# Routed experts in slots of 256 rows, the first product with standing weights

## The chip, the cores and the metric

The kernel runs on one core of a Trainium2 chip. The metric is the device time of one execution, in microseconds, as the median of three executions. A core has five instruction streams that run side by side and meet at semaphores: TensorE (PE in the profile; its weight loads are shown apart as PEld), VectorE (DVE), ScalarE (ACT), GpSimd (POOL) and SyncE (SP, which only issues DMAs here). "Product" below means a chain of matmuls that add up in one place of PSUM, TensorE's result memory of eight banks.

## What is computed

Three stages follow one another: attention whose keys and queries must share a hash bucket, a gated feed-forward layer, and a layer of eight experts of which every row uses one. The change touches the third:

```python
N, D, E, F = (1536, 512, 8, 1024)
logits = x @ w_gate
e_idx = np.argmax(logits, axis=1)
...
for e in range(E):
    mask = e_idx == e
    ...
    h = np.maximum(x[mask] @ w1[e], 0.0)
    ye = h @ w2[e]
    out[mask] = gate_w[mask, None] * eom[mask, e, None] * ye
```

The inputs are drawn from a fixed seed. Counted with the reference on seed 0, the eight experts get 175, 179, 189, 226, 155, 205, 226 and 181 rows.

## The kernel before

All products are made of fp32r matmuls (float32 data in TensorE's faster format) on operands split in a high and a low part: high x high, high x low and low x high are added up, three matmuls for each block of 128 in the contraction. A matmul has a standing operand, 128 x 128, which a weight load puts into the array, and a moving operand, here of up to 512 columns, which streams through.

**Up to the experts** nothing is in another place after the change: attention by pairs of heads, the gated layer (L923), its output projection (L1059, twelve row tiles of 128) and, between the tiles' matmuls, the routing: logits, the chosen expert, the rank of each row among those of its expert, and the row's destination `dest`. POOL scatters each tile of `x2` with an indirect DMA (L797) into a DRAM scratch `routed`, in which two experts share a region and fill it from both ends. The scratch is filled with empty rows beforehand by `fill`, 52 DMAs of 257 KB from SP's queue.

**Slots.** The expert stage works through up to 19 slots of 128 rows (`SLOTS`); 12 are certain (`USED`), the others are run or skipped by a branch on the table entry `in_use`. Which expert a slot belongs to, where its rows lie (`tile_i`), when an expert's weights must be split (`wanted`) and on which of two sides of `expert_w` they lie (`expert_side`) stand in tables that DVE works out after the last tile (L1750 to L1791), and that the engines read with TENSOR_LOAD (`entry`, L350).

**One slot on TensorE** (`step` of the tensor block): `up_half` twice (L1109), each a product of 12 matmuls in which the turned rows `rowsT_h`, `rowsT_l` stand and 512 columns of the weights `w1_h`, `w1_l` move, so that the hidden rows come out with rows on the partitions. DVE applies the relu (L1797) and puts them in `hid`. For the second product the hidden values must have their columns on the partitions, so TensorE turns `hid` in two halves of four 128 x 128 transposes (`turn_hid`, L1120), ACT rounds them to the high part `hidT_h` (L1372) and DVE makes the low part `hidT_l` (L1809). `down` (L1129) is 24 matmuls in two halves, `hidT` standing and 512 columns of `w2` moving. The second product of slot s-1 runs behind the first product of slot s, with the turns between its halves. The next slot's rows (`rows_in`, 257 KB, loaded on ACT's queue at L1360) are turned in the same place (`turn_rows`, L1093), rounded by ACT (L1366) and split by DVE (L1802). `rows_done` (L1380) scales the finished rows into `rows_out`, and POOL stores them to their place in the output with an indirect DMA (L805).

**Weights.** Each expert's 4 MB come in four pieces of 1 MB (`load_piece`, SP's queue, L545 and L548). ACT writes the high part (L1348) and DVE the low part (L1654) of each piece into the side of `expert_w` that is not in use; a piece buffer is loaded again when its low part is done.

**Before the first slot** PE runs `keep_warm` (transposes of the identity into an idle bank, L985) while it waits for the scattered rows.

Of the kernel before, what the change touches and what calls it, by code (L numbers as in the profile page):

```python
# [17 lines left out]
P128 = 128  # L18
# [14 lines left out]
def build(nc, q, k, v, proj, w_gate, w_val, w_out, rms_g, router, out_gate, w1, w2, out):  # L33
# [22 lines left out]
    SLOTS = (N - (E - 1)) // P128 + 1 + (E - 1)  # L56
    USED = -(-N // P128)
    PIECE = C * FE // 2
    ROW = DM + 2
    REGION = NT + 1  # L60
    TILES = E // 2 * REGION
    FILLS = 8
    assert 6 * FILLS < TILES < 7 * FILLS
# [9 lines left out]
    routed_v = routed.rearrange("(s p) n -> p s n", p=P128)  # L73

# [3 lines left out]
    with ExitStack() as ctx:  # L78
# [31 lines left out]
        slot_i = at("slot_i", [P128, SLOTS], I32)  # L110
        slot_f = at("slot_f", [P128, SLOTS], F32)
# [17 lines left out]
        full_at = at("full_at", [1, NT], F32)  # L129
        over = at("over", [1, E, NT], F32)  # L130
        ends = [at(f"ends{i}", [1, 2 * E], F32) for i in range(4)]
        total_i = at("total_i", [1, 3], I32)
        past = at("past", [1, SLOTS, E], F32)
        before_e = at("before_e", [1, SLOTS, E], F32)
        expert_f = at("expert_f", [1, SLOTS], F32)
        expert = at("expert", [1, SLOTS], I32)
        expert_side = at("expert_side", [1, SLOTS], I32)
        odd = at("odd", [1, SLOTS], I32)
        odd_f = at("odd_f", [1, SLOTS], F32)
        nth = at("nth", [1, SLOTS], F32)  # L140
        tile_f = at("tile_f", [1, SLOTS], F32)
        tile_i = at("tile_i", [1, SLOTS], I32)
        change = at("change", [1, SLOTS], F32)
        wanted = at("wanted", [1, SLOTS], I32)
        in_use = at("in_use", [1, SLOTS + 1], I32)
        ended = at("ended", [1, SLOTS + 1], I32)
        stores = at("stores", [1, 2], I32)
        wanted_side = at("wanted_side", [1, SLOTS], I32)
# [100 lines left out]
        hid = at("hid", [P128, FE], F32, offset=addr[0] - 2 * C * P128 * 4)  # L249
        rows_in = [None] * 3 + [at("rows_in3", [P128, ROW], F32)]  # L250
        assert addr[0] <= x2_offset
        addr[0] = xT_offset + 4 * C * FE * 4
        for i in range(3):
            rows_in[i] = at(f"rows_in{i}", [P128, ROW], F32)
        assert addr[0] <= hT_offset - 3 * PIECE * 4
        addr[0] = hT_offset - 3 * PIECE * 4
        for i in range(3):
            piece[i] = at(f"piece{i}", [P128, PIECE], F32)
        addr[0] = x2_offset
        hidT_h = [at(f"hidT_h{i}", [P128, CF, P128], F32R) for i in range(2)]  # L260
        hidT_l = [at(f"hidT_l{i}", [P128, CF, P128], F32R) for i in range(2)]
        rowsT_h = at("rowsT_h", [P128, C, P128], F32R)
        rowsT_l = at("rowsT_l", [P128, C, P128], F32R)
        rows_out = [at(f"rows_out{i}", [P128, DM], F32) for i in range(2)]
# [10 lines left out]
                 "half_ready x_done pool_passed sp_passed "  # L275
# [3 lines left out]
                 "table_made scattered w1_high w2_high w1_low w2_low rows_turned rowsT_high rowsT_low hid_made relu_made hid_turned "  # L279
                 "hidT_high hidT_low "  # L280
                 "out_made outs_ready slots_done").split()
# [4 lines left out]
         half_ready, x_done, pool_passed, sp_passed,  # L286
# [5 lines left out]
         relu_made, hid_turned, hidT_high, hidT_low,  # L292
         out_made, outs_ready, slots_done) = (sems[n] for n in names)
# [58 lines left out]
        def if_used(eng, s_, body):  # L352

            if s_ < USED:
                body()
            elif s_ < SLOTS:
                used = entry(eng, in_use, s_, 1)
                with eng.If(used != 0):
                    body()

        def if_ended(eng, s_, body):

            if s_ >= USED:
                with eng.If(entry(eng, ended, s_, 1) != 0):
                    body()

        def where_wanted(eng, s_, split):

            e = entry(eng, wanted, s_, E - 1)
            with eng.If(e != 0):  # L370
                split(e, entry(eng, wanted_side, s_, 1))
# [1489 lines left out]
```

## Time and profile before

| | |
|---|---|
| median of 3 runs | 803.07 us (802.38 to 803.78) |
| profiled execution | 803.83 us, of it 801.9 us are the span of the trace |
| PE busy | 772.8 us, 96% of the span |
| DVE, ACT, POOL busy | 504.0, 375.3, 317.5 us |
| expert stage, first matmul of the first product to the last scaling of rows | 587.94 to 794.66 us |

Times in the trace are microseconds from the start of the span. A group of instructions is shown as line, engine, operation, out<-in by the program's names, and a count. In square brackets stands how long the engine was idle before it and what ended that. The chain of waits is the work that ended last, followed back from the end: each piece of it is released by the one before. A matmul's shown duration reaches beyond the start of the next one, because they are pipelined; how fast they follow one another is read from the starts, or from a piece of the chain divided by its count.

### The profile page before, as it was taken

The page shows a single profiled execution, that of the slowest core. Times are in us where ns is not written, and L with a number is a line of the kernel's source. Part 1 is how long each engine was busy: PE and PEld are TensorE (multiplying, and loading weights), DVE is VectorE, ACT ScalarE, POOL GpSimd, SP SyncE. Part 2 cuts the span into 40 slices and gives each one's busy share as a digit, 9 for nine tenths or more (in the row PEclk, how much of TensorE's full clock was granted, in tenths as well). Part 3 has the DMA queues.
Part 4 walks back from the last instruction along what each step waited for, and adds up shares of the span by engine and source line. Part 5 has one row for each costly group of instructions (what it writes and reads, how often), then busy time and mean ns, then how long its engine had stood idle before and what let it go on. Part 6 is the DMA issues. An engine that isn't in the chain of part 4 may idle for free.

```text
span 801.9 us, 14327 instructions
## 1 busy us (share of the span) xinstructions
PE 772.8 (96%) x4294; PEld 685.5 (85%) x4294; DVE 504.0 (63%) x983; ACT 375.3 (47%) x672; POOL 317.5 (40%) x340
## 2 busy tenths in 40 slices
PE   7999999999999899999999999999889999999995
PEld 5899889988888899999999988888768888777774
DVE  7999999999987544334343533464673647655640
ACT  5888888888886111110111234434423524553331
POOL 7877777788888353244222001111200201010110
PEclk9999999999999899999999999999999999999999
DMA  6898769657302231112110131031544466454410
GB/s 199 235 236 215 205 166 281 178 142 167 84 2 60 64 89 40 39 39 60 58 39 0 39 121 38 27 132 45 178 146 145 151 228 243 150 203 173 145 47 22
DMA packets 53717, 96.84 MB, mean 121 GB/s; under 512 B 6841, under 2 KB 21189, under 8 KB 53656
## 3 DMA queue, kind: packets, MB, share of 16 engines
q1 hardware_dynamic: 48648, 84.90, 35.7%
q10 hardware_dynamic: 2768, 4.87, 2.3%
q0 software_dynamic: 2240, 6.31, 2.0%
q8 instruction: 32, 0.52, 0.3%
q14 instruction: 29, 0.24, 0.1%
HBM read 58.51 MB, written 21.04 MB: 99 GB/s over the span
## 4 chain that ended last, share of the span: by engine, by line
PE 83%; DVE 10%; issue 3%; ACT 2%; POOL 1%; DMA 1%; ACTq 0%; POOLq 0%; DVEq 0%
PE ps_t L1059 13%; PE ps_s L923 12%; PE ps_t L1129 11%; PE ps_s L1109 11%; PE ps_t L923 6%; PE ps_t L876 6%; DVE pT_l L1483 3%; PE ps_o L923 3%; PE ps_p L923 3%; PE ps_s L862 3%; PE ps_s L863 3%; DVE negmax L1465 2%; PE ps_s L1120 2%; PE ps_o L891 1%; PE ps_o L893 1%
## 5 line engine op out<-in xcount | busy, mean ns | idle before, releaser
L697 POOL TENSOR_SCALAR probs<-probs,rden,alone 128x768 f32<-128x768 f32 x96 | 93.5, 987 | 35.6 <-DVE rden L1477 35.6
L1483 DVE TENSOR_TENSOR pT_l<-ps_t,pT_h 128x384 fp32r<-128x384 f32 x192 | 97.5, 548 | 5.6 <-ACT pT_h L1219 4.6
L805 POOL DMA_INDIRECT out_dram<-rows_out,rows_in x16 | 23.0, 1440 | 193.9 <-ACT rows_out L1380 183.9
L923 PE MATMUL ps_s<-xn,w_h 128*128 128x384 f32 x384 | 97.4, 334 | 0.0
L1209 ACT ACTIVATE probs<-ps_s,negmax 128x768 f32<-128x768 f32 x96 | 87.0, 906 | 19.2 <-DVE negmax L1465 18.5
L1465 DVE TENSOR_REDUCE negmax<-ps_s 128x1 f32<-128x770 f32 x96 | 90.8, 947 | 3.8 <-PE ps_s L863 3.0
L1219 ACT ACTIVATE pT_h<-ps_t 128x384 fp32r<-128x384 f32 x192 | 85.2, 491 | 16.6 <-PE ps_t L876 15.5
L1654 DVE TENSOR_TENSOR expert_w<-piece,expert_w 128x2048 f32 (+1 forms) x32 | 72.1, 2288 | 31.7 <-ACT expert_w L1348 26.4
L876 PE MATMUL ps_t<-ident,probs 128*128 128x128 f32 x576 | 87.4, 282 | 4.5 <-DVE pT_l L1483 2.4
L1109 PE MATMUL ps_s<-expert_w,rowsT_h 128*128 (+1 forms) x256 | 81.9, 401 | 2.7 <-issue 1.6
L1129 PE MATMUL ps_t<-expert_w,hidT_h 128*128 (+1 forms) x256 | 82.1, 402 | 2.2 <-DVE hidT_l L1809 1.4
L876 PEld LDWEIGHTS ps_t<-ident,probs 128*128 128x128 f32 x576 | 63.2, 140 | 24.0 <-DVE pT_l L1483 9.7
L797 POOL DMA_INDIRECT routed<-x,dest x12 | 21.0, 1754 | 128.4 <-DVE x L1732 128.4
L923 PEld LDWEIGHTS ps_s<-xn,w_h 128*128 128x128 f32 x384 | 69.4, 188 | 0.0
L862 PE MATMUL ps_s<-k_a,q_a 128*128 128x384 f32 x192 | 65.8, 343 | 3.5 <-ACT probs L1209 2.1
L1348 ACT ACTIVATE expert_w<-piece 128x2048 f32 (+1 forms) x32 | 59.6, 1907 | 17.4 <-issue 17.4
L1372 ACT ACTIVATE hidT_h<-ps_s 128x512 fp32r<-128x512 f32 x32 | 19.0, 594 | 101.6 <-PE ps_s L1120 73.3
L863 PE MATMUL ps_s<-k_b,q_b 128*128 128x384 f32 x192 | 65.5, 341 | 0.0
L923 PE MATMUL ps_s<-xn,w_l 128*128 128x384 f32 x192 | 64.1, 334 | 0.0
L1059 PE MATMUL ps_t<-wo_h,hs_h 128*128 128x512 f32 x144 | 59.3, 412 | 0.0
L1109 PEld LDWEIGHTS ps_s<-expert_w,rowsT_h 128*128 128x128 f32 x256 | 46.9, 188 | 13.7 <-issue 2.3
L1129 PEld LDWEIGHTS ps_t<-expert_w,hidT_h 128*128 128x128 f32 x256 | 46.7, 188 | 13.8 <-issue 4.0
(252 smaller groups left out, 1719.7 us busy)
## 6 DMA issues: line engine op xcount, KB each, us to landing
piece<-in_moe_w_dram SPq DMA_DIRECT2D x32, 1024.0 KB, 6.1
routed<-filler SPq DMA_DIRECT2D x52, 257.0 KB, 4.3
k_a<-qk_h SPq DMA_DIRECT2D x28, 192.0 KB
rows_in<-routed ACTq DMA_DIRECT2D x17, 257.0 KB, 2.7
rawv<-in_v_dram SPq DMA_DIRECT2D x8, 384.0 KB, 5.9
w_raw<-in_moe_w_gate_dram SPq DMA_DIRECT2D x12, 256.0 KB, 3.1
w_raw<-in_moe_w_val_dram SPq DMA_DIRECT2D x12, 256.0 KB, 3.5
wo_raw<-in_moe_w_out_dram SPq DMA_DIRECT2D x12, 256.0 KB, 2.7
```

The lines of the kernel that those rows point to most:

```text
L697: nc.gpsimd.tensor_scalar(pr, pr, rden[:, j:j + 1], alone[:, j:j + 1], ALU.mult, ALU.add).then_inc(norm_done, 1)
L862: nc.tensor.matmul(o, q_a[par][:, r, queries], k_a[par][:, r, keys], start=True, stop=False)
L863: mm = nc.tensor.matmul(o, q_b[par][:, r, queries], k_b[par][:, r, keys], start=False, stop=True)
L876: mm = nc.tensor.transpose(ps_t[kt % 2][:, i * P128:(i + 1) * P128], probs[:, 3 * g + i, kt * P128:(kt + 1) * P128], ident[:])
L923: mm = nc.tensor.matmul(unit_banks[tg][w][:, 0:G], a_[par][:, w, c, :], xn_at(tg, part, c), start=(n == 0), stop=(n == 3 * C - 1))
L1059: mm = nc.tensor.matmul(ps_t[par][:], a_[par][:, f, :], b_[:, f, :], start=(f == 0 and n == 0), stop=(f == NF - 1 and n == 2))
L1109: mm = nc.tensor.matmul(ps_s[0][:, half, :], a_[:, c, :], b_[:, e_side, c, cols], start=(n == 0), stop=(n == 3 * C - 1))
L1129: mm = nc.tensor.matmul(ps_t[1][:], a_[n % 2][:, c, :], b_[:, e_side, c, :], start=(c == 0 and t == 0), stop=(c == CF - 1 and t == 2))
L1209: nc.scalar.activation(probs[:, j].rearrange("p (a n) -> p a n", a=2), third(ps_s[j % 2]), ACT.Exp, bias=negmax[:, j:j + 1], accum_out=psu ...
L1219: nc.scalar.activation(pT_h[u % 4][:], ps_t[kt % 2][:, 0:G], ACT.Copy).then_inc(high_ready, 1)
L1465: nc.vector.tensor_reduce(negmax[:, c], with_floor(ps_s[j % 2]), AX.XY, ALU.max, negate=True).then_inc(max_done, 1)
L1483: nc.vector.tensor_tensor(pT_l[u % 4][:], ps_t[kt % 2][:, 0:G], pT_h[u % 4][:].bitcast(F32), ALU.subtract).then_inc(low_ready, 1)
```

## The change

A slot now has 256 rows, and eight slots are fixed to the eight experts: slot s is expert s, its side is `(s + 1) % 2` and the first block of its rows is a constant. More than 256 rows of an expert go to up to five extra slots (`extra_slots`), nested branches behind the eighth slot, for which a smaller table is worked out by DVE after its work of slot 0.

In the first product the weights `w1` stand and the 256 turned rows move. The hidden values so come out with their columns on the partitions, as the second product needs them: `hid`, `relu` and `turn_hid` are gone; ACT applies the relu as it rounds (`ACT.Relu`), and DVE takes the larger of the value and zero and subtracts the high part in one instruction. The first product of a slot is 96 matmuls of 256 columns into four banks, the second 2 x 24 of 512 columns into one bank for each half of the rows. The second product follows the first of the same slot; `turn_rows` of the next slot stands between its halves, with a bank for each half.

Rows are loaded 256 at a time (514 KB) into three buffers, those of slot 0 from SP's queue instead of ACT's. The scratch has 56 tiles, so four more are filled. The diff, cut to its core:

```diff
-    SLOTS = (N - (E - 1)) // P128 + 1 + (E - 1)
-    USED = -(-N // P128)
+    ROWS = 2 * P128
+    EXTRA = (N - 1) // ROWS
-    REGION = NT + 1
-    TILES = E // 2 * REGION
+    REGION = N // ROWS + 1
+    BLOCKS = E // 2 * REGION
+    TILES = 2 * BLOCKS
...
+        hid_banks = (ps_s[0][:, 0, :], ps_s[0][:, 1, :], ps_s[1][:, 0, :], ps_s[1][:, 1, :])
+        row_banks = (ps_t[0], ps_o)
+        out_banks = (ps_t[1], ps_p)
...
+            sp.wait_ge(scattered, 16 * NT)
+            sp.dma_start(rows_in[0][:], blocks_v[:, first_block(0)]).then_inc(rows_loaded[0], 16)
-            with sp.Fori(2, E) as e:
+            for e in range(2, E):
                 for k in range(4):
                     load_piece(e, k)
...
-            def up_half(s_, e_side, half):
-                wait(pe, relu_made, 2 * s_ + half - 1)
-                cols = slice(half * 512, half * 512 + 512)
-                n = 0
-                for c in range(C):
-                    for a_, b_ in ((rowsT_h, w1_h), (rowsT_h, w1_l), (rowsT_l, w1_h)):
-                        mm = nc.tensor.matmul(ps_s[0][:, half, :], a_[:, c, :], b_[:, e_side, c, cols],
-                                              start=(n == 0), stop=(n == 3 * C - 1))
-                        n += 1
-                mm.then_inc(hid_made, 1)
-
-            def turn_hid(s_, half):
-                wait(pe, relu_made, 2 * s_ + half + 1)
-
-                wait(pe, hidT_low, 2 * s_ + half - 1)
-                for c in range(4):
...
+            def turn_rows(s_):
+                pe.wait_ge(rows_loaded[s_ % 2], 16 * (s_ // 2 + 1))
+                for half in range(2):
+                    wait(pe, rowsT_low, 2 * (s_ - 1) + half + 1)
+                    for c in range(C):
+                        mm = nc.tensor.transpose(row_banks[half][:, c * P128:(c + 1) * P128],
+                                                 rows_in[s_ % 3][:, half, c * P128:(c + 1) * P128], ident[:])
+                    mm.then_inc(rows_turned, 1)
+
+            def up(s_, side):
+                pe.wait_ge(w1_low, 2 * s_ + 2)
+                pe.wait_ge(rowsT_low, 2 * s_ + 2)
+                for b in range(HB):
+                    wait(pe, hidT_low, HB * (s_ - 1) + b + 1)
+                    for i in range(CF // HB):
+                        f = (CF // HB * b + i) * P128
+                        n = 0
+                        for c in range(C):
+                            for a_, b_ in ((w1_h, rowsT_h), (w1_h, rowsT_l), (w1_l, rowsT_h)):
+                                mm = nc.tensor.matmul(hid_banks[b][:, i * ROWS:(i + 1) * ROWS],
+                                                      a_[:, side, c, f:f + P128], b_[:, c, :],
+                                                      start=(n == 0), stop=(n == 3 * C - 1))
+                                n += 1
+                    mm.then_inc(hid_made, 1)
+
+            def down(s_, half, side):
+
+                wait(pe, outs_ready, 2 * (s_ - 1) + half + 1)
+                for c in range(CF):
+                    pe.wait_ge(hidT_low, HB * s_ + c // (CF // HB) + 1)
...
+            def slot(s_):
+                if s_ >= E:
+                    turn_rows(s_)
+                up(s_, side_of(s_))
+                pe.wait_ge(w2_low, 2 * s_ + 2)
+                down(s_, 0, side_of(s_))
+                if s_ < E - 1:
+                    turn_rows(s_ + 1)
+                down(s_, 1, side_of(s_))
 
             keep_warm(idle_bank, 36)
-            turn_rows(0, 0)
+            turn_rows(0)
             keep_warm(idle_bank, 10)
...
+            def hidT(s_, b):
+                act.wait_ge(hid_made, HB * s_ + b + 1)
+                nc.scalar.activation(hidT_h[:, chunks_of(b), :].rearrange("p c n -> p (c n)"), hid_banks[b],
+                                     ACT.Relu).then_inc(hidT_high, 1)
...
+            def low_hidT(s_, b):
+                dve.wait_ge(hidT_high, HB * s_ + b + 1)
+                nc.vector.scalar_tensor_tensor(hidT_l[:, chunks_of(b), :].rearrange("p c n -> p (c n)"), hid_banks[b], 0.0,
+                                               hidT_h[:, chunks_of(b), :].rearrange("p c n -> p (c n)").bitcast(F32),
+                                               ALU.max, ALU.subtract).then_inc(hidT_low, 1)
```

**TensorE, behind the first product of slot 0.** Before: the last matmuls of the product, the turns of `hid` and of the next slot's rows, then the first product of slot 1, whose matmuls get their side of the weights from a register (the ISA rows).

```order
L1109 MATMUL ps_s<-expert_w,rowsT_h 128x512 x2
L1109 MATMUL ps_s<-expert_w,rowsT_l 128x512
L1120 MATMUL ps_s<-ident,hid 128x128 x4
L1093 MATMUL ps_t<-ident,rows_in_189 128x128 x4
L1120 MATMUL ps_s<-ident,hid 128x128 x4
L30 ISA
L1109 ISA
L1109 MATMUL ps_s<-expert_w,rowsT_h 128x512
```

After, at the same place: the last matmuls of the first product, now of 256 columns, and directly the second product of the same slot.

```order
L1118 MATMUL ps_s<-rowsT_h,expert_w 128x256 x2
L1118 MATMUL ps_s<-rowsT_l,expert_w 128x256
L1118 MATMUL ps_s<-rowsT_h,expert_w 128x256
L1130 MATMUL ps_t<-expert_w,hidT_h 128x512 x2
L1130 MATMUL ps_t<-expert_w,hidT_l 128x512
```

What moved: the two groups of `hid` transposes are gone, and the turns of the rows stand between the halves of the second product.

**VectorE, behind the routing of the last tile.** Before: the end of the tables, then the low parts of expert 1's first piece, of slot 0's rows and of expert 1's second piece.

```order
L1789 SCALAR_TENSOR_TENSOR change<-expert_f,change 1x19
L1790 CAST wanted<-change 1x19
L1791 TENSOR_SCALAR wanted_side<-wanted 1x19
L1654 TENSOR_TENSOR expert_w<-piece_191,expert_w 128x2048
L1802 TENSOR_TENSOR rowsT_l<-ps_t,rowsT_h 128x512
L1654 TENSOR_TENSOR expert_w<-piece_192,expert_w 128x2048
L1797 TENSOR_SCALAR hid<-ps_s 128x512 x2
```

After: one instruction of the tables, both pieces, the rows in two halves, and the four banks of hidden values.

```order
L1702 TENSOR_TENSOR count_f<-ps_s,way 1x8
L1615 TENSOR_TENSOR expert_w<-piece_183,expert_w 128x2048
L1615 TENSOR_TENSOR expert_w<-piece_184,expert_w 128x2048
L1734 TENSOR_TENSOR rowsT_l<-ps_t,rowsT_h 128x4x128
L1734 TENSOR_TENSOR rowsT_l<-ps_o,rowsT_h 128x4x128
L1740 SCALAR_TENSOR_TENSOR hidT_l<-ps_s,hidT_h 128x512 x4
```

What moved: the tables stand behind DVE's work of slot 0, and expert 1's second piece stands ahead of the rows.

**ScalarE, one slot in the middle (slot 1).** After, from the first bank of hidden values to the scaling of the slot's first half of rows:

```order
L1338 ACTIVATE hidT_h<-ps_s 128x512
L1322 ACTIVATE expert_w<-piece_183 128x2048
L1338 ACTIVATE hidT_h<-ps_s 128x512
L1328 DMA rows_in_179<-routed 128x2x514
L1322 ACTIVATE expert_w<-piece_184 128x2048
L1338 ACTIVATE hidT_h<-ps_s 128x512 x2
L1322 ACTIVATE expert_w<-piece_185 128x2048
L1322 ACTIVATE expert_w<-piece_176 128x2048
L1344 ACTIVATE rows_out_182<-ps_t,rows_in_181 128x512
```

Before, in a slot that brings a new expert, both `w1` pieces stand ahead of the slot's first hidden values:

```order
L1348 ACTIVATE expert_w<-piece_191 128x2048
L1348 ISA
L1348 ACTIVATE expert_w<-piece_192 128x2048
L370 UNCONDITIONAL_BRANCH
L1372 ACTIVATE hidT_h_194<-ps_s 128x512
L1366 ACTIVATE rowsT_h<-ps_t 128x512
```

What moved: each piece now stands behind a bank of hidden values, and no register or branch is read between them.

## Rows read from the trace of the kernel before

**Rows 1.** The page: busy time by engine.

```profile
PE 772.8 (96%) x4294; PEld 685.5 (85%) x4294; DVE 504.0 (63%) x983; ACT 375.3 (47%) x672; POOL 317.5 (40%) x340
```

**Rows 2.** The chain of waits, one slot of 128 rows: start, duration, engine, out, line.

```profile
609.16 5.60 PE ps_s L1109 x24
614.76 2.80 PE ps_t L1129 x12
617.56 0.44 PE ps_s L1120 x4
618.00 0.44 PE ps_t L1093 x4
618.43 2.80 PE ps_t L1129 x12
621.24 0.44 PE ps_s L1120 x4
```

**Rows 3.** The chain of waits, gaps at the start and the end of the stage.

```profile
595.23 1.17 issue
...
786.89 0.45 PE ps_s L1120 x4
...
788.76 5.87 PE ps_t L1129 x24
...
794.66 0.69 ACT rows_out L1380
...
795.91 0.29 POOLq L350
```

**Rows 4.** PE in order of time, gated layer, 384 moving columns: start, duration.

```profile
300.21 0.51 PE L923 MATMUL ps_t<-xn,w_h 128*128 128x384 f32 x2
...
300.73 0.33 PE L923 MATMUL ps_t<-xn,w_h 128*128 128x384 f32 x1
```

**Rows 5.** Weight loads in order of time, behind matmuls of 16 moving columns.

```profile
481.87 0.19 PEld L1059 LDWEIGHTS ps_t<-wo_h,hs_h 128*128 128x128 f32 x1
481.98 0.19 PEld L1059 LDWEIGHTS ps_t<-wo_l,hs_h 128*128 128x128 f32 x1
```

**Rows 6.** The engines in order of time, from the last scatter to the first product.

```profile
579.25 0.96 POOL L797 DMA_INDIRECT routed<-x,dest  x1 [3.64 <-DVE x L1732]
...
582.37 3.94 ACTq L1360 DMA_DIRECT2D rows_in<-routed  x2
...
585.16 0.66 PE L1093 MATMUL ps_t<-ident,rows_in 128*128 128x128 f32 x4 [1.19 <-DMA rows_in<-routed]
...
586.36 0.60 ACT L1366 ACTIVATE rowsT_h<-ps_t 128x512 fp32r<-128x512 f32 x1 [5.08 <-PE ps_t L1093]
...
587.12 0.67 DVE L1802 TENSOR_TENSOR rowsT_l<-ps_t,rowsT_h 128x512 fp32r<-128x512 f32 x1
...
587.94 0.48 PE L1109 MATMUL ps_s<-expert_w,rowsT_h 128*128 128x512 f32 x1 [1.04 <-DVE rowsT_l L1802]
```

**Rows 7.** The page: DMAs, KB each and median time from issue to landing.

```profile
piece<-in_moe_w_dram SPq DMA_DIRECT2D x32, 1024.0 KB, 6.1
...
rows_in<-routed ACTq DMA_DIRECT2D x17, 257.0 KB, 2.7
```

**Rows 8.** The page: groups of instructions, busy time and mean ns of one.

```profile
L1654 DVE TENSOR_TENSOR expert_w<-piece,expert_w 128x2048 f32 (+1 forms) x32 | 72.1, 2288 | 31.7 <-ACT expert_w L1348 26.4
...
L1348 ACT ACTIVATE expert_w<-piece 128x2048 f32 (+1 forms) x32 | 59.6, 1907 | 17.4 <-issue 17.4
L1372 ACT ACTIVATE hidT_h<-ps_s 128x512 fp32r<-128x512 f32 x32 | 19.0, 594 | 101.6 <-PE ps_s L1120 73.3
```

**Rows 9.** Stretches about the last tile: length, PE busy, granted clock.

```profile
573.00:577.00 4.00, 2.42 (x18) 1.00 0.31 113
577.70:581.10 3.40, 3.15 (x18) 0.50 0.10 37
```

**Rows 10.** DMA issues of SP in order of time, the fill of the scratch.

```profile
203.94 1.98 SPq L474 DMA_DIRECT2D routed<-filler  x4
```

## Prediction: what the change does to the time

> **What bounds the kernel now.** I read the busy times of the page first, then the chain of waits in the expert stage, then PE in order of time. PE is busy 96% of the span, the next engine 63% [rows 1], so the time is TensorE's row of instructions plus the gaps in it. In the expert stage the chain never leaves PE for a whole slot: the six pieces of [rows 2] add up to 12.52 us, and nothing stands between them. The reader should see three paces there. 24 matmuls of 512 columns take 5.60 us, 0.2333 us each. Twelve take 2.80, the same. Four transposes take 0.44, so 0.109 to 0.11 each. ACT and DVE are busy about half as long as PE here, and what they cost counts only where it ends a PE wait.
>
> The stage goes from the first matmul of the first product at 587.94 [rows 6] to the last scaling of rows at 794.66 [rows 3]: 206.7 us. Its content: 16 slots, since 768 matmuls of 512 columns (48 in a slot, by 0.2333: 179.2 us), and 48 groups of four transposes (32 of `hid`, 16 of rows) by 0.44: 21.1 us. Together 200.3. The other 6.4 us are gaps: 1.2 us before slot 1, where the turned rows and tables of slot 0 had not come through [rows 3]; 1.4 us before the very last product, from 787.34 to 788.76, where ACT and DVE make its operands [rows 3]; and 3.8 us in small pieces about the register reads and branches of the later slots.
>
> **Part 1, TensorE's work.** The columns that stream through are the same: 96 x 256 for 256 rows, where 2 x 24 x 512 stood. The second product is unchanged, 48 matmuls by 0.2333 for 256 rows. Removed: 32 groups of `hid` transposes by 0.44, 14.1 us, all on the path. Turned rows: 56 transposes behind the first slot (8 for each of seven slots), 6.1 us, where 16 groups (7.0 us) stood; the one that goes turned a slot that is not run.
>
> The term on which all hangs is the pace p of a matmul of 256 columns, of which there are 768 in place of 384 of 512. No row shows one. The bounds are its neighbours. From 300.21 to 300.73 three matmuls of 384 columns start, 0.173 us each [rows 4]. At the full clock of 2.4 GHz 384 columns stream in 0.160 us, so 0.013 are added; at 512 columns 0.213, so 0.020 are added [rows 2]. On 256 columns (0.107) that gives 0.120 to 0.127. From below a weight load bounds it: two loads in a row start 0.11 us apart, where the matmuls before them are too short to hide them [rows 5], and turns of 128 columns run at the same 0.11 [rows 2]. A straight line through the two wide rows gives 0.113. So p lies in 0.111 to 0.127, and I take 0.120, because 384 columns are the nearest row in width: 92.2 us for the 768, where 384 by 0.2333 are 89.6. The new form so costs 2.6 us and saves the 14.1.
>
> Each matmul still has a load of its own, twice as many in the first product, and 0.11 us of load lies under 0.120 us of stream; the cover is thin but there. [Rows 4] show the load wholly hidden at 0.173: added to the stream it would have given 0.27. The Trainium skill, page "TensorE: Matmul & The Clock Gate", section "Back-to-back issue gap", has 262 cycles for 256 columns, 0.109 us, and 128 columns / 1.2 GHz for a load in "LDWEIGHTS", 0.107 us; by it the sum would be 8 us lower. For 512 columns it has 0.216, and the trace shows 0.233, so the measurement decides against it.
>
> **Part 2, gaps inside the stage.** The wait before slot 1 and the one before the last product go, because `hid` has no way over DVE and back to PE any more: ACT reads the bank that PE wrote. What is late next? The second product starts on bank 0, three banks old. It needs bank 3 only after 18 matmuls, 4.2 us, and ACT 0.59 [rows 8] plus DVE 0.67 (as `rowsT_l` [rows 6]) plus some 0.6 us of handing over are 1.9. The register reads and branches also go; the eight slots are straight code. The turned rows of the next slot have 5.6 us (`down` of the second half) for two ACT and two DVE instructions, but behind them on the queues stand the two `w2` pieces: ACT 2 x 1.91, DVE 2 x 2.29 [rows 8]. Counted from the end of the first product, DVE has bank 3 at 1.9, the pieces at 6.5 and the rows at 8.4, and PE wants them at 5.6 + 0.9 + 5.6 = 12.1 us. In a slot ACT has 4 x 0.59 + 4 x 1.91 + 2 x 0.59 + 2 x 0.69 = 12.6 us of work and DVE 4 x 0.67 + 4 x 2.29 + 2 x 0.67 = 13.2, of 23.7. A piece is asked for at about 8 us of the slot before, when DVE has made the low part out of its buffer, lands in 6.1 [rows 7], and is wanted at 3 us of the next slot: 13 us of cover. DVE's 20 table steps of slot 0 (some 4 us) end before slot 1's second bank. All these cost nothing. I leave 1.0 us for gaps that I do not see, 0.4 of it the end of the last matmul.
>
> Stage: 92.2 + 89.6 + 6.1 + 1.0 = 188.9 us, 17.8 less than 206.7.
>
> **Part 3, the start.** The rows of slot 0 are wanted by an idle PE: the last scatter is issued at 579.25, the load at 582.37, PE turns at 585.16 and the product starts at 587.94 [rows 6]. The load has 514 KB now. Between 257 KB in 2.7 us and 1024 KB in 6.1 [rows 7] a straight line puts it at 3.8: 1.1 us later. It stands on SP's queue ahead of expert 2's first piece, which may take bandwidth from it: up to 1 us more. Then two halves follow each other through PE, ACT and DVE: the second is turned 0.44 later [rows 2], ACT's second is done some 0.5 later than one was, DVE's follows; before, DVE was held 0.15 us by a piece [rows 6]. I take +0.5. The tables that leave the queue of DVE give nothing, since the rows were later than they. So +1.6 us, between 0.5 and 3.5. PE's clock stood at 0.50 for 3.4 us from 577.7, behind a stretch in which PE was busy 2.4 of 4 us with narrow work [rows 9]; the longer wait may call for it again, as the first product starts. Such a stretch would cost half its length, 1.7 us, and lies in the range.
>
> **Part 4, costs of nothing.** Four more fills are issued by SP behind 203.94 in some 2 us [rows 10]; the next weights behind them on SP are wanted when PE comes to the gated layer, more than 30 us on. At the end SP reads one table entry behind the last store, some 0.3 us as POOL's [rows 3]. POOL's own ending ran longer than SP's, so 0 to 0.5; I take 0.
>
> **Sum.** -17.8 + 1.6 = -16.2 us. The profiled execution took 803.83, 1.93 outside its span and 0.76 above the median of 803.07; on the median the forecast is 786.9 us.
>
> **The rivals.** (A) *The weight load comes out from under the shorter matmul; slower.* It sits in `up`, in each of 768 matmuls, and decides from p = 0.120 + 16.2/768 = 0.141 us on. For it: two loads at 0.11 leave 0.01 us of slack, and no row has 256 columns. Against: a narrower matmul should not be slower than one of 384, so 0.173 is the end: 768 x 0.053 = 40.7 us, 827.6 us. Up to here 5%. If a load could not overlap a running matmul at all, p would be 0.11 + 0.107 = 0.217 and the kernel 74 us slower than forecast, 861; [rows 4] contradict it by 0.173 against 0.27, and I leave it 1%. (The Trainium skill, same page, section "The mechanism", says that a load overlaps matmuls in flight only where it goes to other rows of the array; all here go to the same.) All of A: 6%.
>
> (B) *A smaller gain by a wait for each slot.* PE stops before `down` or before the next `up`, because ACT's strict order (rows behind pieces, pieces behind DMA) is later than I add up: with 1 us in each of eight slots 795 us. For it: pieces, rows and stores share the DMA queues, and the small gaps of the later slots of before may have another cause than branches. Against: 2.3 us of slack at the tightest place. 10%.
>
> (C) *The pace is the load's.* p = 0.111: 6.9 us less, 780.0 us. For it: the line through the wide rows. 8%.
>
> (D) *The slots are not fixed as meant*: an expert with over 256 rows needs an extra slot, with its weights and rows loaded in the open, some 40 us more, 827 us. By the counts of the reference the largest has 226 rows; 1%.
>
> **How the numbers follow.** The forecast's case (p of 0.118 to 0.127, start as in part 3) has 75%: 784 to 794. A 6% and D 1% end above 803. C and B reach 780 to 796. The range 781.5 to 795 leaves out A, D, the tail of B and the deepest part of C, some 18% together. What lies over 0.2% from the median (1.6 us, about what a measurement of this kernel can tell) on the fast side: 92%; same 1%, slower 7%.
>
> **What would show it.** In the profile after: 24 matmuls of 256 columns in 2.9 us; the chain on PE with pieces of the first product of 11.5 us and of the second of 5.6; no `hid`; slots 23.7 us apart; no PE wait above 0.5 us between slots; the first product 1.6 us later than 587.94. Wrong, if the 96 matmuls take over 13.5 us, if PE waits for DVE's `hidT_l` or `rowsT_l` in each slot, or if the first product starts behind 591.5.

## Result and profile after

| | before | after |
|---|---|---|
| median | 803.42 us (4 executions, 802.38 to 804.17) | 782.54 us (4 executions, 782.19 to 783.52) |
| profiled execution | 803.83 us, span 801.9 | 782.19 us, span 780.4 |
| expert stage, first product to last scaling | 587.94 to 794.66: 206.7 us | 587.29 to 774.51: 187.2 us |
| one pair of 128-row slots, one 256-row slot | 25.04 us | 23.48 us |

The ratio of after to before is 0.9748, with a 95% interval of 0.9734 to 0.9761: faster, by 20.9 us. 786.9 us was forecast, between 781.5 and 795.0. The direction and the range held. The gain was larger than forecast by 4.7 us, and where those come from is the question for the runs.

The page of after, which answers [rows 1] and the `rows_in` line of [rows 7]: busy time by engine, the first product's group, the rows' load.

```profile
PE 754.2 (97%) x4546; PEld 688.1 (88%) x4546; DVE 481.5 (62%) x935; ACT 376.4 (48%) x671; POOL 310.0 (40%) x340
...
L1118 PE MATMUL ps_s<-rowsT_h,expert_w 128*128 128x256 f32 x512 | 92.5, 281 | 0.6 <-DVE rowsT_l L1734 0.6
...
rows_in<-routed ACTq DMA_DIRECT2D x7, 514.0 KB, 3.8
```

The chain of waits of after from the last scatter through one whole slot, which answers [rows 2] and [rows 6]: start, duration, what.

```profile
577.68 3.03 DMA routed<-x,dest
...
580.73 3.76 DMA rows_in<-routed
...
584.53 0.67 PE ps_t L1104 x4
...
585.23 0.61 ACT rowsT_h L1333
...
585.86 1.30 DVE rowsT_l L1734 x2
...
587.29 11.63 PE ps_s L1118 x96
598.92 5.59 PE ps_t L1130 x24
604.51 0.44 PE ps_t L1104 x4
604.95 0.44 PE ps_o L1104 x4
605.39 5.61 PE ps_p L1130 x24
611.00 11.39 PE ps_s L1118 x96
```

From 587.29 on each piece starts where the one before it ended. The slot is 11.39 + 5.6 + 0.88 + 5.6 us of TensorE and nothing else. 11.39 over 96 matmuls is 0.1186 us for one: that is the pace p on which the forecast hung. The end of the chain, which answers [rows 3], and then all waits of PE from 577 us to the end (line waited for, total, times, longest):

```profile
751.87 11.39 PE ps_s L1118 x96
763.26 5.61 PE ps_t L1130 x24
768.87 5.62 PE ps_p L1130 x24
...
774.51 0.70 ACT rows_out L1344
```

```profile
PE ps_t L1104 <- DMA rows_in<-routed: 2.3, 1, 2.3
PE ps_s L1118 <- DVE rowsT_l L1734: 0.6, 1, 0.6
```

Both waits belong to slot 0. The gap of 1.2 us before the second slot and that of 1.4 us before the last product [rows 3] have no counterpart.

The two spans differ by 21.5 us. Cut at the last scatter, the first product and the last scaling, in the two profiled executions:

| | before | after | measured | forecast |
|---|---|---|---|---|
| start of the span to the last scatter | 579.25 | 577.68 | -1.6 | 0 |
| last scatter to first product | 8.69 | 9.61 | +0.9 | +1.6 |
| expert stage | 206.7 | 187.2 | -19.5 | -17.8 |
| last scaling to the end of the span | 7.2 | 5.9 | -1.3 | 0 |

### The profile page after: what moved, and what is told of

The parts are those of the page before. It is cut to its first block, busy times and chain, and to the rows that moved or that the text cites. A ratio compares the mean times of both kernels' runs of the same rounds, so it can differ in the third digit from the quotient of the medians.

```text
span 780.4 us, 13334 instructions
## 1 busy us (share of the span) xinstructions
PE 754.2 (97%) x4546; PEld 688.1 (88%) x4546; DVE 481.5 (62%) x935; ACT 376.4 (48%) x671; POOL 310.0 (40%) x340
## 4 chain that ended last, share of the span: by engine, by line
PE 82%; DVE 9%; issue 3%; POOL 2%; ACT 2%; DMA 2%; ACTq 0%; POOLq 0%; DVEq 0%
PE ps_t L1070 13%; PE ps_s L934 12%; PE ps_s L1118 12%; PE ps_t L934 6%; PE ps_t L887 6%; PE ps_t L1130 6%; PE ps_p L1130 6%; DVE pT_l L1444 4%; PE ps_o L934 3%; PE ps_p L934 3%; PE ps_s L874 2%; PE ps_s L873 2%; DVE negmax L1426 2%; PE ps_o L902 1%; PE ps_o L904 1%
## 5 line engine op out<-in xcount | busy, mean ns | idle before, releaser
L1118 PE MATMUL ps_s<-rowsT_h,expert_w 128*128 128x256 f32 x512 | 92.5, 281 | 0.6 <-DVE rowsT_l L1734 0.6
L816 POOL DMA_INDIRECT out_dram<-rows_out,rows_in x16 | 15.8, 985 | 182.6 <-ACT rows_out L1344 182.6
L1615 DVE TENSOR_TENSOR expert_w<-piece,expert_w 128x2048 fp32r<-128x2048 f32 x32 | 72.6, 2290 | 15.1 <-ACT expert_w L1322 15.0
L1118 PEld LDWEIGHTS ps_s<-rowsT_h,expert_w 128*128 128x128 f32 x512 | 79.2, 189 | 1.1 <-issue 0.8
L1118 PE MATMUL ps_s<-rowsT_l,expert_w 128*128 128x256 f32 x256 | 71.9, 281 | 0.0
L1740 DVE SCALAR_TENSOR_TENSOR hidT_l<-ps_s,hidT_h 128x512 fp32r<-128x512 f32 x32 | 22.0, 689 | 71.5 <-ACT hidT_h L1338 71.5
L1322 ACT ACTIVATE expert_w<-piece 128x2048 fp32r<-128x2048 f32 x32 | 60.2, 1906 | 0.0
L1070 PE MATMUL ps_t<-wo_h,hs_l 128*128 128x512 f32 x144 | 56.4, 392 | 0.0
```

What stands on the lines that cost most here:

```text
L1070: mm = nc.tensor.matmul(ps_t[par][:], a_[par][:, f, :], b_[:, f, :], start=(f == 0 and n == 0), stop=(f == NF - 1 and n == 2))
L1118: mm = nc.tensor.matmul(hid_banks[b][:, i * ROWS:(i + 1) * ROWS], a_[:, side, c, f:f + P128], b_[:, c, :], start=(n == 0), stop=(n == 3 * ...
```

## Experiments

The kernel before ran beside each group of these kernels; its median was 802.69 us both times (14 and 9 executions). Ratios are against it.

**1. Fixed slots alone.** The kernel before with 16 slots of 128 rows, two for each expert; expert, side and tile are constants, and tables and branches are gone. The products, and the turns of `hid`, are those of before.

```diff
-    SLOTS = (N - (E - 1)) // P128 + 1 + (E - 1)
-    USED = -(-N // P128)
+    SLOTS = USED = 2 * E
...
-                if s_ == 0:
-                    return 0, 1
-                return entry(pe, expert, s_, E - 1), entry(pe, expert_side, s_, 1)
+                return s_ // 2, (s_ // 2 + 1) % 2
...
-                t = 0 if isinstance(s_, int) and s_ == 0 else entry(act, tile_i, s_, TILES - 1)
+                e = s_ // 2
+                t = REGION * (e // 2) + (s_ % 2 if e % 2 == 0 else REGION - 1 - s_ % 2)
```

> The kernel before, with its 16 slots of 128 rows fixed to the experts (two each) by constants, and without the tables, register reads and branches; TensorE's matmuls and transposes are all as before, but for the turned rows of the slot that is not run. Theory (the gaps of the stage were register reads, branches and the wait for the tables, some 5.0 us of the 6.4; the 1.4 us before the last product stay, and so do the 14.1 us of hid turns): 5.4 us less than before, 798.0 us, range 796.8 to 799.2. Rival (the gaps come from DMA traffic or instruction fetch and stay whatever the code is): at most 1.5 us less, 801.9 or more. In the profile the theory wants slots of 12.5 us throughout and no idle time of PE between them.

Measured: 800.66 us (799.68 to 802.09, 10 executions), ratio 0.9975 (0.9962 to 0.9988). That is above the range. In the stage the small gaps did go: every slot from the third on took 12.52 us. But the stage, 591.30 to 794.42, is 203.1 us, 3.6 less than before, where the theory wanted 5.4: the gap before the second slot stayed (1.06 us), though there are no tables. And the first product started at 591.3 instead of 587.9. The engines in order of time, then the chain of waits:

```profile
582.32 0.39 SPq L539 DMA_DIRECT2D piece<-in_moe_w_dram  x1
582.58 0.84 ACTq L1352 DMA_DIRECT2D rows_in<-routed  x2
```

```profile
582.58 5.78 DMA rows_in<-routed
...
588.40 1.11 PE ps_t L1086 x4
589.52 2.05 PE ps_s L978 x10
591.57 5.59 PE ps_s L1100 x24
```

A weight piece of 1024 KB was issued 0.26 us ahead of the rows, and the rows needed 5.78 us instead of 2.8 [rows 6]. In before, DVE worked on the tables from 579.0 to 585.0, so the low part of the piece, and with it the next load into its buffer, came late: the piece was issued at 587.37. The tables had kept the DMA queues clear for the rows. Four transposes then took 1.11 us in place of 0.67, since PE was granted 0.50 of its clock (1.2 GHz) after the longer wait, for 3.4 us from 587.9. That the load beside it is what slowed the rows is only argued from this run; the fifth run tests it.

**2. The turns put back in number.** The changed kernel, in which the transposes of the next slot's rows are made three times over in seven slots: 112 transposes more, to no other use.

```diff
-                    for c in range(C):
+                    for c in range(C * (3 if s_ else 1)):
+                        c = c % C
```

> The changed kernel, in which TensorE makes each of the turns of rows three times from slot 1 on: 112 transposes more (7 x 16), nearly the 128 that the change removed, at a place where nothing waits for them. Theory (the time is TensorE's row of instructions, and every transpose of it costs 0.109 us): +12.2 us, 794.8 us, range 794.2 to 795.6. Rival (a part of them lies under a wait for ACT, DVE or DMA that PE has anyway): +6 us or less, under 789.

Measured: 796.05 us (795.02 to 797.79, 5 executions), ratio 0.992 (0.9896 to 0.9945): 13.5 us more than the changed kernel, where 12.2 were expected; that is 0.4 us above the range. Chain of waits, in one slot:

```profile
605.64 1.31 PE ps_t L1105 x12
606.96 1.31 PE ps_o L1105 x12
```

1.31 for 12 is 0.109 us each, and the first product to the last scaling, 588.42 to 787.88, is 12.2 us longer than in after; the rest of the 13.5 lies outside the stage (in this profile the last scatter came 1.4 us later than in after). A transpose between the products costs its full time on the path; 128 of them less are the 14.1 us of the forecast.

**3. The first product in matmuls of 128 columns.** 1536 of them instead of 768 of 256; each with a weight load of its own.

```diff
-                        for c in range(C):
-                            for a_, b_ in ((w1_h, rowsT_h), (w1_h, rowsT_l), (w1_l, rowsT_h)):
-                                mm = nc.tensor.matmul(hid_banks[b][:, i * ROWS:(i + 1) * ROWS],
-                                                      a_[:, side, c, f:f + P128], b_[:, c, :],
+                        for h in range(2):
+                            n = 0
+                            for c in range(C):
+                                for a_, b_ in ((w1_h, rowsT_h), (w1_h, rowsT_l), (w1_l, rowsT_h)):
+                                    mm = nc.tensor.matmul(hid_banks[b][:, i * ROWS + h * P128:i * ROWS + (h + 1) * P128],
+                                                          a_[:, side, c, f:f + P128], b_[:, c, half_cols(h)],
```

> The changed kernel, first product in 1536 matmuls of 128 moving columns instead of 768 of 256; the sums are the same. Theory (a weight load needs 0.11 us and is hidden only as far as columns stream; at 128 columns it is the bound): pace 0.110 us, 1536 x 0.110 - 768 x 0.1186 = +77.9 us, 860.4 us. Rival (a matmul costs its columns plus a fixed 0.013 us, loads never show): pace 0.066 us, +10.3 us, 792.8 us. A load that does not overlap at all would give 0.16 us a matmul and over 930 us.

Measured: 865.0 and 885.5 us, two executions, of which the second was profiled. PE in order of time in the profiled one, a stretch of PE (length, PE busy, granted clock, DMA share, GB/s), and one of all engines (PE, PEld, DVE, ACT and POOL busy, then the same):

```profile
650.13 0.39 PE L1119 MATMUL ps_s<-rowsT_h,expert_w 128*128 128x128 f32 x2
650.36 0.28 PE L1119 MATMUL ps_s<-rowsT_l,expert_w 128*128 128x128 f32 x1
650.47 0.39 PE L1119 MATMUL ps_s<-rowsT_h,expert_w 128*128 128x128 f32 x2
```

```profile
640.00:660.00 20.00, 20.00 (x165) 1.00 0.41 151
```

```profile
584.90:632.70 47.80, 46.98 (x216) 46.52 (x217) 4.15 (x6) 4.98 (x7) 0.00 (x0) 0.50 0.15 55
```

At full clock three matmuls take 0.34 us (650.13 to 650.47), 0.111 to 0.113 each; at half clock 0.64, from 600.18 to 600.82 in the same view, 0.213 each. From 256 to 384 columns a matmul's pace grows by 0.054 us (0.1186, and 0.173 in [rows 4]), so the 128 columns alone would allow about half of 0.111; here the pace is no longer that of the stream: it is the 0.11 us at which two weight loads follow one another [rows 5]. That agrees with the first theory. At 256 columns the same load lies under 0.1186 us, with less than 0.01 us to spare. The surprise is the clock: the grant stayed at 0.50 for 47.8 us from 584.9, while PE was busy for 47.0 us of it. The execution to compare is the other one: 865.0 us is 82.5 us above the changed kernel, where 77.9 were expected and the rival had 10.3. Of these, 80.0 are the first products: at full clock the chain has 21.39 us for the 192 matmuls of a slot, in place of 11.39 for 96. It is a single execution without a profile.

**4. The last bank made late.** The changed kernel with the two `w2` pieces ahead of the fourth bank of hidden values, on ACT and on DVE (the diff shows ACT's part).

```diff
                 hidT(s_, 2)
-                hidT(s_, 3)
                 if ahead:
                     for k in (2, 3):
                         split_piece(s_ + 1, k, side_of(s_ + 1))
+                hidT(s_, 3)
```

> The changed kernel, with the two w2 pieces of the next expert ahead of the last bank of hidden values on ACT and on DVE, instead of behind it. Work is the same on every engine. Theory (the order on ACT and DVE is free as long as bank 3 is ready 18 matmuls after the first product ends, 15.6 us into the slot; by the durations DVE is through with it at 16.6): PE waits about 1.1 us in each of seven slots, +7.7 us, 790.2 us, range 788 to 793. Rival (the chain has more slack than added up, as the pieces were early in any case): no change, under 783.5.

Measured: 789.04 us (788.01 to 789.45, 4 executions), ratio 0.9824 (0.9797 to 0.9852), 6.5 us more than the changed kernel. The waits of PE's weight loads:

```profile
PEld ps_t L1130 <- DVE hidT_l L1740: 7.0, 7, 1.0
```

Seven waits, one in each slot that has pieces to split. A weight load is wanted a little ahead of its matmul, so the path loses less than the 1.0 us shown: the first product to the last scaling, 588.42 to 781.50, is 5.9 us longer than in after, 0.84 us a slot. So the slack behind which the changed kernel hides the fourth bank is real and small: two pieces ahead of it use it up. It is the order of ACT's and DVE's work that keeps rival B out, not a lack of work on them.

**5. Fixed slots with the rows alone.** The first kernel, and SP issues expert 2's first piece only when slot 0's rows have landed.

```diff
             load_piece(1, 3)
+            sp.wait_ge(rows_loaded[0], 16)
             with sp.Fori(2, E) as e:
```

> e1 (the kernel before with its 16 slots fixed), with one wait more on SP: expert 2's first piece is not asked for until slot 0's rows have landed. Theory (e1 lost at the start what it gained in the slots: without the tables the 1 MB piece is asked for 0.26 us ahead of the rows, which then took 5.8 us to land instead of 2.8, and a stretch of half clock fell on the start): the rows land in 2.8 us, the first product starts by 588.3, 3.5 us less than e1, 797.1 us, range 796.2 to 798.2. Rival (the rows were late for another reason): e1's 800.7 us again.

Measured: 796.14 us (795.8 to 798.69, 4 executions), just under the low end of the range, ratio 0.9926 (0.9905 to 0.9948), 4.5 us less than without the wait. The engines in order of time, then the chain:

```profile
580.69 0.84 ACTq L1353 DMA_DIRECT2D rows_in<-routed  x2
...
583.68 4.46 SPq L539 DMA_DIRECT2D piece<-in_moe_w_dram  x2
```

```profile
580.69 2.65 DMA rows_in<-routed
...
583.39 0.67 PE ps_t L1087 x4
...
584.08 0.61 ACT rowsT_h L1359
...
585.55 5.83 PE ps_s L1101 x24
```

The rows land in 2.65 us, and no low clock follows. The price of the collision is shown: of the 4.5 us, 3.1 are the landing, and 0.7 lie between PE's turn and the product (2.90 us in the first run, 2.16 here), where the lower clock slowed the turns. The other 0.7 is not placed. This kernel also splits the gain. Fixed slots, with nothing changed in the products, are worth 6.5 us of the 20.9; the other 14 come with the slots of 256 rows and the missing turns (15.9 us less of stage, 1.6 us more of start). Its stage is 585.55 to 788.63, 203.1 us, 3.6 less than before (0.44 of it the turned rows of a slot that is not run), and it keeps the gap before the second slot (1.05 us from 592.82) and the one before the last product (1.3).

**6. The rows on ACT's queue.** The changed kernel, in which ACT issues the load of slot 0's rows and SP's pieces do not stand behind it.

```diff
-            sp.wait_ge(scattered, 16 * NT)
-            sp.dma_start(rows_in[0][:], blocks_v[:, first_block(0)]).then_inc(rows_loaded[0], 16)
...
+            act.wait_ge(scattered, 16 * NT)
+            act.dma_start(rows_in[0][:], blocks_v[:, first_block(0)]).then_inc(rows_loaded[0], 16)
             rowsT(0)
```

> The changed kernel with one part undone: slot 0's rows are loaded on ACT's queue again, and SP asks for expert 2's pieces as soon as their buffers are free. Theory (rows and pieces then share the DMA engines, as in e1): the 514 KB land in about 6.5 us instead of 3.8, and half clock may be granted at the start; +2.7 to +4 us, 786.0 us, range 785 to 787.5. Rival (the place of the load is no matter, since the pieces come later or on other rings): 782.5 us, under 783.5.

Measured: 786.26 us (784.77 to 786.65, 4 executions), ratio 0.9795 (0.9778 to 0.9812), 3.7 us more than the changed kernel. The chain:

```profile
580.49 5.84 DMA rows_in<-routed
...
586.37 1.11 PE ps_t L1102 x4
...
590.18 11.40 PE ps_s L1116 x96
```

The piece was issued at 580.09, the rows at 580.49: 5.84 us again. In the changed kernel the piece stands behind the rows on one queue, and the rows take 3.76. The move of the load to SP's queue, which the forecast took for a risk (a piece right behind it "may take bandwidth from it"), is what protects it. Queue and order change together here; rows ahead of the piece but on another queue were not tried.

**7. An attempt at a faster version.** The rows come as two halves of 257 KB from ACT's and SP's queues, SP holds the pieces back until its half has landed, and at the end SP reads the table before it waits for the last stores.

```diff
-            sp.dma_start(rows_in[0][:], blocks_v[:, first_block(0)]).then_inc(rows_loaded[0], 16)
+            sp.dma_start(rows_in[0][:, 1], blocks_v[:, first_block(0), 1]).then_inc(rows_loaded[0], 16)
+            sp.wait_ge(rows_loaded[0], 16)
...
+            act.wait_ge(scattered, 16 * NT)
+            act.dma_start(rows_in[0][:, 0], blocks_v[:, first_block(0), 0]).then_inc(rows_first, 16)
```

> The changed kernel, its start and end shortened: slot 0's rows come in two loads of 257 KB, the first half on ACT's queue and the second on SP's, each with a semaphore of its own; SP asks for expert 2's first piece when the second half has landed; and SP reads the table entry for the extra slots ahead of its wait for the last stores. Theory: the first half lands in 2.9 us instead of 3.8, so the first product starts 0.9 us earlier, and SP's 1.3 us at the end (only 0.3 us longer than GpSimd's) go: -1.2 us, 781.3 us, range 780.5 to 782.2. Rival (two loads at once land no earlier than one of both halves, and GpSimd's ending sets the end): -0.3 us or less, 782.2 to 782.8.

Measured: 782.85 us (782.12 to 783.16, 5 executions), ratio 0.9752 (0.9738 to 0.9766): as the changed kernel, and not the 781.3 us of the theory. The chain, and one stretch of it (PE, PEld, DVE, ACT and POOL busy, granted clock, DMA share, GB/s):

```profile
580.14 3.81 DMA rows_in<-routed
...
584.00 0.66 PE ps_t L1113 x4
...
587.12 12.05 PE ps_s L1127 x96
```

```profile
585.10:588.50 3.40, 3.40 (x18) 3.40 (x17) 1.29 (x2) 0.67 (x2) 0.00 (x0) 0.50 0.89 353
```

The two halves landed 3.6 and 3.8 us after their issue, with no piece beside them, as late as one load of 514 KB ahead of a piece. So the piece behind the rows costs the changed kernel nothing, and halving the load won nothing. A stretch of half clock then came as the product began, and the 96 matmuls took 12.05 us. The end hardly moved: 5.7 us from the last scaling to the end of the span, where after has 5.9. SP's read of the table did not set it.

**8. The kernel before once more**, for one profile.

> The kernel before, unchanged, for a second profile. Two things stand apart by 1.5 us each in the profiles of before and after in places where the code is the same: a stretch of half clock about 264 us (6.8 us long against 3.4), and the last store (4.3 us from issue to landing against 2.8, with one DMA engine busy with instruction fetches). If both belong to the one execution they differ here too; if they belong to the code of before, they are here again: 6.8 us at half clock and a last store over 4 us. I expect the first to vary and the second to be here again, since the skipped slots' branches fetch code at the end.

Measured: 805.18 us, span 803.2. Its last store took 3.8 us from issue to landing. What moved on the DMA queues in a stretch of 1.6 us that begins 0.9 us behind the issue of that store, and then in after in the same stretch behind its own last store:

```profile
## 3 DMA queue, kind: packets, MB, share of 16 engines
q0 software_dynamic: 75, 0.10, 16.6%
q8 instruction: 1, 0.02, 4.8%
q14 instruction: 1, 0.01, 2.1%
issues: line engine op xcount, KB each, median us to landing
out_dram<-rows_out,rows_in POOLq DMA_INDIRECT x1, 3.8
```

```profile
## 3 DMA queue, kind: packets, MB, share of 16 engines
q0 software_dynamic: 80, 0.26, 42.3%
```

In after all 80 packets of the store move in it. In before 75 of 80 do, though they hold fewer bytes (0.10 MB against 0.26); in the first profile of before the other five came up to 1.2 us after such a stretch. The DMA engines meanwhile carry a fetch of instructions: 4.8% of 16 engines over 1.6 us would be 1.2 us on one of them (queue q8), and 2.1% would be 0.5 us (q14). The store landed in 4.3 and 3.8 us in the two profiles of before, in 3.2 us in the second run, and in 2.7 or 2.8 us in after and in the six others. The end behind the last scaling was 6.7 us here and 7.2 in the first profile, so it varies by half a microsecond in one kernel; over 4 us were expected for the store again, and it took 3.8. The stretch of half clock did vary, as expected: 3.4 us long here, from 267 us on.

## Why the prediction was right, and where its sizes were off

**Direction.** The bound was read rightly: one row of TensorE, in which a slot has no wait. The second run put 112 turns in and the stage grew by their full time, so turns taken out come off it; and matmuls of half the width cost 1.8 us more for the same columns (91.4 against 89.6).

**Part 1, the pace.** p was taken as 0.120 us and is 0.1186, so the first product takes 91.4 us instead of 92.2. The neighbour in width was the right row to lean on, the straight line (0.113) the worse one. The whole stage adds up without a rest: 11.63 + 7 x 11.39 = 91.4 us, 16 halves of the second product by 5.61 are 89.8, and 7 x 0.88 of turns 6.2, together 187.3 before rounding, against 187.2 measured. The bound from below was the right one too: the third run gives 0.111 where the load sets the pace, and rival C needed that at 256 columns. Rival A would have needed 0.141, and a load that cannot overlap a running matmul 0.217. The Trainium skill, page "TensorE: Matmul & The Clock Gate", section "LDWEIGHTS", has 128 columns / 1.2 GHz, 0.107 us, for a load; the 0.111 us of the third run agree within 4%. The 0.109 us for 256 columns of "Back-to-back issue gap" are 8% below the 0.1186 measured, and the measurement decides.

**Part 2, the gaps.** 1.0 us was left for gaps that I did not see. There are none (about -1.0 us). The slack for the fourth bank was worked out right in kind: the fourth run spends it and pays 0.84 us a slot. One cause named for the gap before the second slot was wrong: it stays at 1.06 us in a kernel without tables (first run). The forecast did not rest on it.

**Part 3, the start.** +1.6 us was forecast and +0.9 measured, and the step that failed is a sentence: "The tables that leave the queue of DVE give nothing". Against the fifth run, which has fixed slots and rows of 257 KB alone, both terms hold: the rows turn 3.80 us after the load's issue instead of 2.70 (+1.1, as forecast), and from PE's turn to the product it is 2.76 us instead of 2.16 (+0.6, where +0.5 stood). But in before the same two steps took 2.79 and 2.78. The 0.6 us of the second step stood on two queues at once. The chain of waits of before runs over DVE:

```profile
584.84 0.16 DVE wanted_side L1791
585.00 2.19 DVE expert_w L1654
587.19 0.61 DVE rowsT_l L1802
```

The tables ended before the rows were turned, but the low part of a weight piece stood behind them on DVE, and the rows' low part behind that. In after the pieces are out of the way by 582.5:

```profile
578.01 4.49 DVE L1615 TENSOR_TENSOR expert_w<-piece,expert_w 128x2048 fp32r<-128x2048 f32 x2 [0.59 <-ACT expert_w L1322]
```

Under that delay lay one of ACT. It started 1.20 us after PE's turn, and not 0.69 as in the fifth run, because it had slot 1's load to issue first, for which it read the table: the second of the two issues at 582.37 in [rows 6] ends only at 586.31, and ACT starts at 586.36. ACT was done at 586.96, DVE's piece at 587.19. The forecast took DVE's piece at the 0.15 us by which it outlasted ACT, and missed that ACT itself was late by 0.5. With both gone, the second half of the rows cost nothing net: this step took 2.78 us before and 2.76 after, where +0.5 was forecast. The contention of up to 1 us, and the low clock of 1.7 us, did not come.

**Part 4, costs of nothing.** The fills cost nothing that shows. "POOL's own ending ran longer than SP's" was right, but the end of before held 1.3 us that I had not looked for (0.8 in its second profile): the last store landed in 4.3 us, where most other kernels need 2.7. It went with the tables and branches, since the first run (without them, products as before) ends 5.6 us behind its last scaling, and before 7.2. That the instruction fetches beside it are the cause is argued from two profiles; no run takes them away alone.

**The base.** The last 1.6 us of the profiled difference lie ahead of the last scatter, in code that is the same. In the profiled before PE had 0.50 of its clock for 6.8 us about 264 us and for 3.4 about 18; in after 3.4 and none. The second profile of before has 3.4 us at 267, the fourth experiment, a form of the changed kernel, 6.8 at 263. The last scatter came at 579.25 and 579.45 us in the two profiles of before, at 579.59 and 577.55 in the first and fifth runs, which share its code up to there, and between 577.33 and 579.07 in after and the other forms of it. So this differs from execution to execution and is not shown to be work of the change. It is in the profiled pair and in part perhaps in the medians.

**The sum.** From the forecast gain of 16.2 us: pace 0.8 more and gaps 1.0 more, start 0.7, end 1.3, together 20.0. Measured by the medians is 20.9. What remains, 0.9 us, is of the size of the clock's stretches, and no run here settles it.

## What to carry to other kernels

Where one engine's row of instructions is the path, ask which of its instructions only change the layout of a result, and whether the other operand can stand instead; narrowing the stream is cheap only as long as a weight load still hides under it, here at 256 columns (0.1186 us against a load's 0.111) and not at 128. When work is removed from an engine that is not on the path, look at what it was holding back: the buffers that it frees earlier start transfers, and a short urgent load beside a long one lost 2 to 3 us, while put ahead of it on the same queue it lost nothing. When a step goes away, do not ask only when it ended: ask what stood behind it on every engine's queue, and read the end of the span too.

## What the hardware showed that was not expected

- A load of 257 KB took 2.65 us with no weight piece beside it and 5.78 us when a load of 1024 KB on another queue was issued 0.26 us ahead of it; 514 KB took 3.76 us ahead of such a piece on its own queue, and 5.84 us beside one that had started 0.4 us earlier. Two halves on two queues took as long as the whole on one: 3.6 and 3.8 us.
- TensorE's granted clock stayed at 0.50 for 47.8 us under a dense row of 128-column matmuls with a load each, in the one execution of two that was profiled. Shorter stretches, of 3.4 us, came as PE turned the first rows in the first, the sixth and the seventh run, and in the seventh although its rows landed as early as in after, where none came there.
- A last store of some 80 packets landed in 4.3 and 3.8 us where instruction fetches moved in the same 1.6 us, in 3.2 us in the second run, and in 2.7 or 2.8 us in seven other profiles. That the fetches are the cause is not shown.
